# Storing an attention bias on chip: rows four apart and one transfer per half tile, in place of rows eight apart and one transfer per query tile

## What is computed

```
scores = q @ k.T / sqrt(D)                         # B=4, H=8, S=576, D=64
psi_rel = log1p(|i - j|);  psi_i = log1p(max(i, 1))
h = max((psi_rel / psi_i) * w1 + b1, 0)            # hidden = 32
bias = h @ w2                                      # S x S x H, the same for every batch
attn = softmax(scores + bias);  x = attn @ v       # x: 2304 x 512
out = (sigmoid(x @ w_gate) * (x @ w_val)) @ w_out  # d_ff = 1536
```

## Time and profile before

| what | value |
|---|---|
| time, median of 3 runs | 817.29 us (816.87 to 821.43) |
| the profiled execution | 821.9 us |
| its span, first to last instruction | 820.1 us |
| mean granted TensorE clock | 0.990 |
| busy: TensorE, VectorE, ScalarE, GpSimd | 784.1, 332.5, 337.5, 194.1 us |
| packets on the hardware queue | 86272, 49.05 MB |

### The profile page before, as it was taken

How to read it: one execution, slowest core, us unless ns; L and a number is a source line. 1 busy time by engine, 2 the same in 40 slices (tenths; PEclk the granted TensorE clock), 3 DMA queues, 4 the chain that set the end, 5 groups by cost and what they waited for, 6 DMA issues and landing times.

```text
span 820.1 us, 13204 instructions
## 1 busy us (share of the span) xinstructions
PE 784.1 (96%) x5008; PEld 628.1 (77%) x5008; DVE 332.5 (41%) x797; ACT 337.5 (41%) x684; POOL 194.1 (24%) x363
## 2 busy tenths in 40 slices
PE   5676999999999999999989999999999999999998
PEld 2233666666666666669978998999899889989996
DVE  6884666666666666634330221122022202211220
ACT  6885666666666666643321221122122212212210
POOL 0000666647544545668300000000000000000000
PEclk9998999999999999999999999999999999999999
DMA  5778333332342333213322000100010010000001
GB/s 130 176 175 175 75 86 86 79 98 62 76 113 58 73 81 84 63 54 98 116 89 65 1 1 15 62 1 1 26 52 1 14 64 1 1 26 14 1 1 38
DMA packets 86334, 49.89 MB, mean 61 GB/s; under 512 B 60160, under 2 KB 79744, under 8 KB 86272
## 3 DMA queue, kind: packets, MB, share of 16 engines
q1 hardware_dynamic: 86272, 49.05, 22.9%
HBM read 28.98 MB, written 9.44 MB: 47 GB/s over the span
## 4 chain that ended last, share of the span: by engine, by line
PE 84%; DMA 7%; ACT 3%; DVE 2%; POOL 2%; SPq 1%; issue 1%; POOLq 0%; ACTq 0%
PE f_ps L991 18%; PE g_ps L941 16%; PE u_ps L941 15%; PE v_ps L923 10%; PE so_ps L857 10%; PE ty_ps L870 4%; PE tx_ps L882 3%; DMA bias<-bias_rows 3%; PE so_ps L852 2%; DMA w_raw<-in_w_gate 2%; DMA x_raw<-in_w_out 2%; POOL w L510 1%; ACT feats L559 1%; PE so_ps L805 1%; PE tx_ps L899 1%
## 5 line engine op out<-in xcount | busy, mean ns | idle before, releaser
L941 PE MATMUL g_ps<-x_h,w 128*128 128x384 f32 x576 | 146.6, 335 | 1.4 <-DVE hid L774 1.4
L594 ACT ACTIVATE probs<-neg_scores,neg_max 128x576 f32<-128x576 f32 x144 | 110.4, 768 | 87.5 <-DVE neg_max L714 87.5
L941 PE MATMUL u_ps<-x_h,w 128*128 128x384 f32 x576 | 146.3, 334 | 0.0
L774 DVE TENSOR_TENSOR hid<-u_ps,sig 128x384 f32<-128x384 f32 x72 | 40.1, 557 | 244.3 <-PE u_ps L941 244.3
L493 POOL TENSOR_SCALAR probs<-probs,recip 128x512 f32<-128x512 f32 x128 | 88.5, 692 | 186.4 <-DVE recip L728 186.4
L714 DVE CUSTOM_DVE_ANT_0 neg_scores<-so_ps,bias 128x576 f32<-128x576 f32 x128 | 91.9, 756 | 62.8 <-PE so_ps L857 62.8
L941 PEld LDWEIGHTS g_ps<-x_h,w 128*128 128x128 f32 x576 | 103.9, 188 | 2.5 <-DVE hid L774 1.7
L941 PEld LDWEIGHTS u_ps<-x_h,w 128*128 128x128 f32 x576 | 103.9, 188 | 0.5 <-issue 0.5
L655 ACT ACTIVATE h_h<-hid 128x384 fp32r<-128x384 f32 x72 | 37.9, 526 | 149.6 <-DVE hid L774 149.6
L941 PE MATMUL g_ps<-x_l,w 128*128 128x384 f32 x288 | 96.3, 334 | 0.0
L941 PE MATMUL u_ps<-x_l,w 128*128 128x384 f32 x288 | 96.2, 334 | 0.0
(11 more groups left out here) (71 smaller groups left out, 1000.9 us busy)
## 6 DMA issues: line engine op xcount, KB each, us to landing
bias<-bias_rows SPq DMA_DIRECT2D x16, 576.0 KB, 6.5
x_raw<-attn_transposed SPq DMA_DIRECT2D x6, 768.0 KB, 4.7
out<-out_sb SPq DMA_DIRECT2D x18, 256.0 KB, 2.0
q_raw<-in_q SPq DMA_DIRECT2D x32, 128.0 KB, 2.6
k_raw<-in_k SPq DMA_DIRECT2D x32, 128.0 KB, 2.4
v_main<-in_v SPq DMA_DIRECT2D x32, 128.0 KB, 2.3
w_raw<-in_w_gate SPq DMA_DIRECT2D x12, 256.0 KB, 2.9
w_raw<-in_w_val SPq DMA_DIRECT2D x12, 256.0 KB, 2.9
```

What stands on the lines that cost most here:

```text
L594: nc.scalar.activation(probs[s % RING][:, place, :], neg_scores[s % 2][:, place, :], ACT.Exp, bias=neg_max[:, stat(s, place)], scale=-1.0, ...
L774: nc.vector.tensor_tensor(hid[f % 2][:, :], u_ps[f % 3][:, 0:CH], sig[f % 2][:, :], ALU.mult).then_inc(gated, 1)
L941: last = nc.tensor.matmul(bank[f % 3][:, 0:CH], w[:, f, part, i, t, :], x[:, t, :], start=m == 0, stop=m == len(terms) - 1)
```

## The change

ROW_STEP becomes 4. A unit of a main tile now has eight rows in the first 64 rows of the query tile and eight in the second 64, four apart in each half. Since these 16 rows no longer have one step, a duo is stored by two transfers, one for each half, each from 64 partitions of the buffer to 8 rows. Which row a duo begins with is now `tile_row(n)`: 0 to 3, then 32 to 35. In the tail the 16 rows of a unit are four apart over 64 rows, so a transfer takes them all: four transfers for a duo, two for each unit. The window of log distances grows from 1127 to 1139 columns. The counts that the waits use follow.

```diff
-ROW_STEP = 8
+ROW_STEP = 4
+HALF_TILE = P // 2
+TILE_UNITS = P // QU
-TAIL_DMAS = 8
+MAIN_DMAS, TAIL_DMAS = 2, 4
+def tile_row(n):
+
+    return n // ROW_STEP * HALF_TILE // 2 + n % ROW_STEP
...
 def duo(d):
 
-    if d < ROW_STEP:
-        return 0, d
-    if d < ROW_STEP + TAIL_DUOS:
-        return NT, 2 * (d - ROW_STEP)
-    return 2, d - ROW_STEP - TAIL_DUOS
+    if d < TILE_UNITS:
+        return 0, tile_row(d)
+    if d < TILE_UNITS + TAIL_DUOS:
+        return NT, 2 * (d - TILE_UNITS)
+    return 2, tile_row(d - TILE_UNITS - TAIL_DUOS)
...
     if t < NT:
-        return (t + u % 2) * P + at + j * GRP * ROW_STEP
-    return NT * P + at + u % 2 + j % 2 * GRP * ROW_STEP + j // 2 * GRP
+        return (t + u % 2) * P + at + j // 2 * HALF_TILE + j % 2 * GRP * ROW_STEP
+    return NT * P + at + u % 2 + j * GRP * ROW_STEP
...
                 if t < NT:
-                    sp.dma_start(bias[at::ROW_STEP, :, t:t + 2, :], bias_rows[i][:, :, :]).then_inc(bias_stored[i], 16)
+                    for n in range(2):
+                        row = n * HALF_TILE + at
+                        sp.dma_start(bias[row:row + (H - 1) * ROW_STEP + 1:ROW_STEP, :, t:t + 2, :],
+                                     bias_rows[i][n * P // 2:(n + 1) * P // 2, :, :]).then_inc(bias_stored[i], 16)
                     return
                 for e in range(2):
                     for a in range(2):
-                        for n in range(2):
-                            row = (1 - a) * REM + at + e + n * GRP
-                            sp.dma_start(bias_tail[row:row + 7 * ROW_STEP + 1:ROW_STEP, :, :],
-                                         bias_rows[i][n * P // 2 + a:(n + 1) * P // 2:2, e, :]) \
-                                .then_inc(bias_stored[i], 16)
+                        row = (1 - a) * REM + at + e
+                        sp.dma_start(bias_tail[row:row + (QU - 1) * ROW_STEP + 1:ROW_STEP, :, :],
+                                     bias_rows[i][a::2, e, :]).then_inc(bias_stored[i], 16)
```

More of the change, by code:

```diff
@@ L85, in base_row @@
     if t < NT:
-        return (t + u % 2) * P + at + j * GRP * ROW_STEP
-    return NT * P + at + u % 2 + j % 2 * GRP * ROW_STEP + j // 2 * GRP
+        return (t + u % 2) * P + at + j // 2 * HALF_TILE + j % 2 * GRP * ROW_STEP
+    return NT * P + at + u % 2 + j * GRP * ROW_STEP
 def duo_stored(d):
-    return sum(16 * (TAIL_DMAS if duo(n)[0] == NT else 1) for n in range(d % ROW_BUFS, d + 1, ROW_BUFS))
+    return sum(16 * (TAIL_DMAS if duo(n)[0] == NT else MAIN_DMAS) for n in range(d % ROW_BUFS, d + 1, ROW_BUFS))
 def program(nc, q, k, v, hidden_wb, w2_sets, wg, wv, wo, log_dist, inv_log_pos, out):
@@ L707, in shift @@
                     for d in range(ROW_BUFS):
-                        last = max(n for n in range(ROW_STEP if s == 0 else DUOS) if n % ROW_BUFS == d)
+                        last = max(n for n in range(TILE_UNITS if s == 0 else DUOS) if n % ROW_BUFS == d)
                         dve.wait_ge(bias_stored[d], duo_stored(last))
```

## The result

The changed kernel takes 825.29 us (median of 6 runs, 823.79 to 828.51) against 818.45 us before (6 runs, 816.87 to 821.43): ratio 1.0079, 95% interval 1.0058 to 1.0100, some 6.5 us slower. The forecast was 816.0, a gain of 1.2 us. The size is near that of rival 1 (+5.6 us), but not by its pace of 4.05 us for a duo.

What follows compares the result with a forecast made beforehand. TensorE was taken as the bound, busy 96% of 820.1 us; the bias stage's last pair starting 1.15 us earlier gave a sum of -1.2 us, carried to the median 817.29: 816.1, forecast 816.0, range 810 to 826.

Steps and rivals of the forecast that it cites:

- rival 1: Main stores in the bias stage: eight engines keep the tail stores' pace, 4.05 us for a duo; +5.6 us, 822.9; chance 0.18.
- The stage and its waits: Bias stage, 6 to 74.2 us: ScalarE's copies wait 10.4 us for stores, all that faster stores could give back.
- Eight outer rows, eight engines, and the next transfer on the same eight: New main stores: each half uses eight DMA engines, so the halves run one after the other; DMA share about 0.5.
- I take 3.28: Main stores: time for a duo's data on eight engines, at the rate of the load of x; bounds 2.89 to 5.95 us.
- Between duos SP has time (2.94 us for 1.14), so most are free: SP's queue: 16 more main issues at 0.57 us cost nothing, except 0.57 us before the q and k loads.
- Tails: Tail duos 8 and 9: eight fewer issues at 0.60 us; of 1.57 + 0.91 us and the 0.85 lost, 1.4 us gained.
- The loads of v: SP's queue: each lot holds SP some 4 to 5 us and delays the stores of duos 12 and 14.
- Duo 17 ... Free: Last main store, after unit 35: goes from 73.1, lands by 80, is waited for only at 85.13; no cost.
- My sign of a wrong reading: Behind the scores' start: a change of more than 1 us there would make the whole reading wrong.
- A shift is passed on whole: Behind the bias stage: TensorE works without a gap, 736.91 of 745.90 us, so the last pair's shift moves the end equally.
- Rival 2: Every main store: only eight engines, each kept at 12.4 GB/s, 5.95 us for a duo; +37 us, 854; chance 0.15.
- Rival 3: Main stores: the halves run beside each other on different engines, 1.5 to 1.8 us; some 7 us back, 810; chance 0.07.

## Why the prediction was wrong, point by point

- *The stage and its waits.* Right in the main: the change acts on the bias stage's stores, the computation is unchanged, and the start of the last pair moves the scores. Two points below limit it, duo 17 and the shift behind the scores.
- *Eight outer rows, eight engines, and the next transfer on the same eight.* Right, read from the share of 0.52 in the tails: every stretch of main stores has 0.44 to 0.50. Undoing the halves (one transfer, rows four apart) brings share 0.94 and the time of before.
- *"I take 3.28".* This term failed first. It is 3.53 us in the cleanest stretch and 3.35 to 4.15 in the changed kernel. I had named 3.5 us as the point from which the change costs; the measured value is on its other side. But by my own steps 3.53 gives about 0 and not +6.5 us, so put into those steps this term is about 1 us of the miss. A duo that takes longer than its computation does more than that, since the stores pile up: with every load out of the way the eight-row stores still cost 6.6 us. Both ends of my bounds were open because the nearest rows (tails, 4.05) and the ones I leaned to (the load of x, 3.28) differ; the truth was between them, and I had chosen the end that agreed with an argument.
- *"Between duos SP has time (2.94 us for 1.14), so most are free".* This step failed and weighs more: an issue takes 1.07 us, not 0.57, two of them 2.1, and SP's loads stretch as well. The loads of q and k take 8.0 us to issue, not 6.0, so duo 5's store goes at 35.24 and not 33.05, and the copy that waits for it starts at 41.99, not 39.4. My own formula with the measured terms, 35.24 plus 3.05 plus 3.53, gives 41.8: of the 2.6 us 2.2 are SP's queue and 0.25 the pace. At the end it is the same: duo 14's store goes at 70.33, where I had 64.0, lands 6.2 us later, sooner than the 7.7 I had given it, and the last pair starts 4.9 us behind my 71.7. The run with two transfers of sixteen rows shows that the number of issues is not the cause. No term of mine had the issue time grow with what is outstanding.
- *Duos 0 to 4.* I had them free. At 3.35 us against 2.94 they fall behind by some 0.4 us each, and the waits of 0.31, 0.52 and 1.69 us follow, the last with data of the q loads under way beside the store.
- *Tails.* No wait on a tail store, as forecast. I gave the tails 2.25 us (1.4 gained and 0.85 made good), and the kernel with one transfer for a main store, rows four apart and the tail's four transfers did gain 2.3 us by its ratio; in the profiled runs its scores start 3.8 us earlier (70.52, against 74.27), so that the two numbers meet is chance. In the changed kernel the tails are worth 4.2 to 5.5.
- *The loads of v.* SP was held 4.8 and 5.0 us by the two lots, as forecast, and the waits behind them stayed (3.23 us).
- *"Duo 17 ... Free".* Wrong: its second half was issued at 79.76, where I had 73.1 for the store, and landed at 87.4, not by 80; VectorE waited 2.81 us. My sign of a wrong reading, a change of more than 1 us behind the scores' start, did not show in the sum (746.2 against 745.8 us from there to the end), but only because the clock was higher at that start; the wait is such a change.
- *"A shift is passed on whole".* Only while the clock is the same: from the scores' start to the end the kernel before took 745.8 us in its profiled run, at a mean granted clock of 0.990, and with its loads spread 740.6 at 1.000, with the same work and no late store in either. No term of mine had the clock.
- *Rival 1* foresaw the size, +5.6 us against +6.5 or so, by luck: it had a pace of 4.05 with free issues; the pace was better and the issues dearer. *Rival 2* has its nearest relative in the halves with rows eight apart: 5.1 us for a duo and +25 us. *Rival 3*, engines apart for the two halves, is false for SP's queue. From GpSimd's more than eight engines ran and no copy waited, at 807.8; its 1.5 to 1.8 us for a duo were not seen, since the computation asks for one in 2.94.

The Trainium skill's port map (SBUF — State Buffer, "Door 1: The DMA port swizzle") puts the rates in the right order: by it eight rows eight apart in one half reach 4 ports, an estimated 108 GB/s at 27 each, and the run shows 116, somewhat more; sixteen rows, at either step, reach 8, 218, and the runs show 204 to 206. Eight rows four apart reach 8 ports too, but the runs show 142 to 176, so its 2.7 us for a duo was too hopeful. What holds the rate below that was not tried. The rule on which engines a transfer takes (DMA: Bandwidth & Descriptors, "Why a DMA increments its semaphore by 16 and not by 1") says that a transfer on fewer than sixteen engines takes the lowest-numbered ones from SP's and ScalarE's queues and the next in turn from GpSimd's. No trace here has the numbers of the engines, but the shares agree: 0.44 to 0.50 from SP, and 0.58 to 0.76 for GpSimd's queue alone.

## What to carry to other kernels

Before splitting a transfer, look at the outermost dimension of both sides: with 8 there instead of 16, two transfers from SP's queue ran one after the other on the same half of the DMA engines, and the DMA share of a stretch (0.5) tells it. A store that is back to back with others is priced by its time against the computation's, here 3.5 us against 2.94, and when it is the longer one, issues, loads behind it and the last landing all get dearer together. Loads that nobody needs yet belong behind the stores in the queue: that alone gave 0.6% here. One transfer of sixteen rows with all loads out of the way gave 1.1%, and the halves from an idle engine's queue 1.2%. And where TensorE is the bound, compare the granted clock before the times: an earlier start of a stage and a higher clock behind it look alike in the total.

## What the runs showed that I had not expected

- The same two halves, issued by GpSimd, ran on more than eight engines and took every wait for a store away (807.84 us, against 825.29 from SP and 819.40 from SP with the loads out of the way).
- The pace of an engine differed with how far apart the rows of a transfer are, though it moves as many bytes: 14.8 GB/s with rows eight apart, 20.9 with rows four apart (167/8), both on eight engines. On sixteen engines the step made no difference (204 and 206 GB/s).
- The time of an issue on SP is not fixed: 0.57 us in the median before, 1.07 with twice as many transfers on half of the engines.
- The granted clock is part of every time here. From the scores' start to those of the tail step TensorE needs 12.73 us for 60 products in the kernel before (above, clock 0.66) and 8.64 with the halves from GpSimd:

```profile
63.56:74.93 11.37, 8.64 (x60) 5.72 (x60) 7.96 (x25) 6.85 (x17) 6.34 (x13) 1.00 0.68 184
```

  Of the 15.5 us between these two profiled runs (820.1 and 804.6 us) 10.7 lie before the scores and 4.8 behind their start (745.8 against 741.0). The times of one kernel spread the same way: the fastest run of the kernel before beside the last group took 815.2 us at a mean clock of 0.995, the slowest 821.6 at 0.988. What would be left of each difference at one clock was not tried.
